# Last stage of a two-part kernel: a third PSUM buffer for h, the reciprocal in SBUF, and a loop of six blocks

## The chip, the cores and the metric

The kernel runs on one core of a Trainium2 chip. The metric is device time in microseconds, the median of several executions. Lower is better.

## What is computed

The program does two things one after the other. First a long convolution by Fourier transform, `y = irfft(rfft(x * v) * rfft(filter))`, whose result is gated as `x * y`. Then a wide layer with a rational activation on each of the 24,960 rows of that result (128 wide, 2,048 hidden):

```python
h = x @ w_in
P = a[0] + a[1] * h + a[2] * h**2 + a[3] * h**3
Q = 1.0 + abs(b[0]) * abs(h) + abs(b[1]) * h**2
out = (P / (Q + 1e-06)) @ w_out
```

All of it is float32. The change touches only the second part, which is the last stage of the kernel.

## The kernel before, in words

There are three stages. The first transforms `x * v` and the filter along one axis, the second multiplies the spectra and transforms back along the other, and the third, the last, unfolds the result, gates it with `x` and runs the wide layer.

The last stage goes over 30 blocks of 416 tokens for each of two batches. The unit of work is a step: one pair of hidden tiles, 2 x 128 hidden units by 416 tokens, so that most instructions work on 128 partitions by 832 elements. There are 16 steps to a block (`BLOCK_PAIRS`) and 480 in all. Every engine has its own order, written out by hand, and the engines meet only at semaphores. For step q it is:

- TensorE multiplies `g_s` of step q into `acc_p` (L878) and then makes h of step q+6 (`hidden`, L867, `LEAD_H = 6`) in one of two PSUM buffers `h_p`. A buffer is taken again when the numerator two steps earlier has been made.
- ScalarE takes the logarithm of the denominator of step q+1 (L669), the Exp of minus the logarithm of step q, which is the reciprocal and goes to the PSUM tensor `r_p` (L676), and for step q+4 the magnitude of h (L650, even steps only) and the square (L659).
- VectorE makes the magnitude of h of step q+4 on odd steps (L747), then `g_s` of step q out of numerator and reciprocal (`activation`, L785), then the numerator `num` of step q+4 out of the square and h (L752). Both of the last two are scalar_tensor_tensor instructions with two tensor inputs.
- GpSimd makes the denominator less its constant as `slope = mag * b1 + b0` (L617), then `den = slope * mag` (L625), both from SBUF to SBUF.

`num`, `square`, `mag`, `slope`, `den` and `g_s` lie in SBUF. `h_p`, `r_p`, `acc_p` and `m_p` are in PSUM: four banks for the two h buffers, two for `r_p`, one each for the others. The unfolding of the next block, its gating, its two transposes and the split of its values into a high and a low part go in between at the steps named in `UNFOLD`, `TIMES_X`, `TURN_IN`, `SPLIT_HI` and `SPLIT_LO`, all by way of the one bank `m_p`.

The loops are written so that the first and the last turn stand outside, and the turns between them are a hardware loop. A turn is two blocks (32 steps).

One instruction of the first stage matters for the argument. `product` on VectorE (L264, a tensor_tensor) multiplies `x_s` by `v_s`, both in SBUF, once in each of its 30 blocks, while GpSimd subtracts `uh_hi` from `uh` (L211, also a tensor_tensor, twice in each block):

```python
nc.vector.tensor_tensor(uh[:, s, :, 0:BD]..., x_s[:, s], v_s[:, s], ALU.mult)
nc.gpsimd.tensor_tensor(uh_lo[:, s, at], uh[:, s, at], uh_hi[:, s, at].bitcast(F32), ALU.subtract)
```

Other VectorE instructions of that stage that run beside L211 (L283, L285) take one tensor from PSUM (`g_p`) and one from SBUF (`part_s`).

Of the kernel before, what the change touches and what calls it, by code (L numbers as in the profile page):

```python
# [22 lines left out]
I32 = mybir.dt.int32  # L23
ALU = mybir.AluOpType
# [48 lines left out]
def hyena_mlp(nc, x, v, pos_emb, w1, w2, w_in, w_out, a, b, tab, out):  # L73
# [30 lines left out]
    with ExitStack() as whole:  # L104
# [420 lines left out]
        with ExitStack() as ctx:  # L525
# [50 lines left out]

            UNFOLD, TIMES_X, TURN_IN, SPLIT_HI, SPLIT_LO = (2, 6), (3, 7), (3, 7), (5, 9), (5, 9)
            SUMS, TURN_OUT, LEAVE = (0, 8), (0, 12), (2, 14)

            @block.sync  # L580
            def _(sp):
# [14 lines left out]
                load(1, 1)  # L596
                with sp.Fori(0, ITERS - 1) as i:
# [39 lines left out]
            def _(act):  # L637
# [7 lines left out]
                def magnitude(i, q):  # L645
                    G = i * PER + q
                    act.wait_ge(h_done, G + 1)
                    if positive(G - DEEP + 1):
                        act.wait_ge(den_done, G - DEEP + 1)
                    nc.scalar.activation(mag[:, q % DEEP], h_p[:, q % 2, :, 0:TOK], ACT.Abs).then_inc(mag_act, 1)  # L650

                def squared(i, q):
                    G = i * PER + q
                    act.wait_ge(h_done, G + 1)
                    if q % 2:
                        act.wait_ge(mag_dve, i * (PER // 2) + q // 2 + 1)
                    if positive(G - SQUARES + 1):
                        act.wait_ge(num_done, G - SQUARES + 1)
                    nc.scalar.activation(square[:, q % SQUARES], h_p[:, q % 2, :, 0:TOK], ACT.Square, bias=centre[:]  # L659
                                         ).then_inc(square_done, 1)  # L660
# [27 lines left out]
                def step(i, q, more, ahead):  # L688

                    blk, m = i * SLOTS + q // BLOCK_PAIRS, q % BLOCK_PAIRS  # L690
                    if ahead or q + 1 < PER:
# [24 lines left out]
                for q in range(PER):  # L716
                    step(ITERS - 1, q, q < BLOCK_PAIRS, q + LEAD_E < PER)
                c = J_BLOCKS * BATCH - 1
# [5 lines left out]
            def _(dve):  # L724
# [17 lines left out]
                def magnitude(i, q):  # L742
                    G = i * PER + q
                    dve.wait_ge(h_done, G + 1)
                    if positive(G - DEEP + 1):
                        dve.wait_ge(den_done, G - DEEP + 1)
                    nc.vector.tensor_scalar(mag[:, q % DEEP].bitcast(I32), h_p[:, q % 2, :, 0:TOK].bitcast(I32), NO_SIGN, None,  # L747
                                            ALU.bitwise_and).then_inc(mag_dve, 1)

                def numerator(i, q):  # L750
                    dve.wait_ge(square_done, i * PER + q + 1)
                    nc.vector.scalar_tensor_tensor(out=num[:, q % NUMS], in0=square[:, q % SQUARES], scalar=level[:],  # L752
                                                   in1=h_p[:, q % 2, :, 0:TOK], op0=ALU.add, op1=ALU.mult).then_inc(num_done, 1)

# [25 lines left out]
                def activation(i, q):  # L780
# [24 lines left out]
                def step(i, q, more, ahead):  # L805
                    blk, m = i * SLOTS + q // BLOCK_PAIRS, q % BLOCK_PAIRS
                    if m in SUMS:
# [7 lines left out]
                    def side():  # L815
                        nxt, s = (blk + 1) * 2, (q // BLOCK_PAIRS + 1) % SLOTS
                        if more and m in TIMES_X:
                            times_x(nxt + TIMES_X.index(m), i + (q // BLOCK_PAIRS + 1) // SLOTS, s, TIMES_X.index(m))
                        if more and m in SPLIT_LO:
                            split_lo(nxt + SPLIT_LO.index(m), s, SPLIT_LO.index(m))  # L820
# [12 lines left out]
                for q in range(PER):  # L833
                    step(ITERS - 1, q, q < BLOCK_PAIRS, q + LEAD_E < PER)
                sums(J_BLOCKS * BATCH - 1)

            @block.tensor
            def _(pe):
# [18 lines left out]
                def hidden(i, q):  # L857
                    G = i * PER + q
                    if q % BLOCK_PAIRS == 0:
                        pe.wait_ge(lo_done, (i * SLOTS + q // BLOCK_PAIRS + 1) * 2)  # L860
                    if positive(G - 1):
                        pe.wait_ge(num_done, G - 1)
                    s, b_ = q // BLOCK_PAIRS, q // PAIRS % BATCH
                    for t in range(2):
                        at = ((q % PAIRS) * 2 + t) * 128
                        for n, (w, f) in enumerate(((w_lo, xy_hi), (w_hi, xy_hi), (w_hi, xy_lo))):
                            mm = nc.tensor.matmul(h_p[:, q % 2, t, 0:TOK], w[:, at:at + 128], f[:, s, b_, :],  # L867
                                                  start=(n == 0), stop=(n == 2))
                    mm.then_inc(h_done, 1)

                def project(i, q):
                    G = i * PER + q
                    pe.wait_ge(act_done, G + 1)
                    if q % PAIRS == 0 and positive(G):
                        pe.wait_ge(oT_done, i * SLOTS * BATCH + q // PAIRS)
                    for t in range(2):
# [12 lines left out]
                def step(i, q, more, ahead):  # L889
                    blk, m = i * SLOTS + q // BLOCK_PAIRS, q % BLOCK_PAIRS  # L890
                    project(i, q)
# [3 lines left out]
                    if more and m in UNFOLD:  # L895
# [7 lines left out]

                        rows(nxt + half, i + (q // BLOCK_PAIRS + 1) // SLOTS, s, half, freed)
                    if more and m in TURN_IN:
# [26 lines left out]
                for q in range(PER):  # L932
                    step(ITERS - 1, q, q < BLOCK_PAIRS, q + LEAD_H < PER)
                turn_out(J_BLOCKS * BATCH - 1, lambda: pe.wait_ge(o_done, J_BLOCKS * BATCH - 1))
# [21 lines left out]
```

## Time and profile before

| | |
|---|---|
| median of 3 runs | 2239.24 us (2235.86 to 2241.52) |
| the profiled execution's own time | 2240.67 us |
| its span | 2238.9 us |
| TensorE busy | 2048.9 us, 92% |
| VectorE busy | 1805.7 us, 81% |
| ScalarE busy | 1822.0 us, 81% |
| GpSimd busy | 1894.0 us, 85% |
| first and last start of `den` (L625) | 675.1 and 2223.7 us |

The engines are PE (TensorE matmul), PEld (TensorE weight load), DVE (VectorE), ACT (ScalarE), POOL (GpSimd) and SP (the queue that issues the transfers). L625 is line 625 of the kernel. The last stage begins at about 645 us and fills the rest. Busy shares over the whole span mix three stages, so they are to be read stage by stage.

### The profile page before, as it was taken

To read this page: it belongs to the slowest core of one execution; us is meant where nothing else is said; L and a number is where in the kernel's file an instruction comes from. 1 tells how busy PE (TensorE), PEld (TensorE's weight loads), DVE (VectorE), ACT (ScalarE), POOL (GpSimd) and SP (SyncE) were. 2 spreads that over 40 slices of the span, in tenths; PEclk is the share of its full clock that TensorE was granted. 3 is DMA by queue.
4 is the path that set the end of the run, shared out by engine and by line. 5 is a ranking of instruction groups with operands and counts; after the bars stand their busy time and mean duration, and the time that the engine had idled before them with its cause. 6 is when DMAs were issued, how large, how long until landed. Compare 5 with 4: busy or idle time off the path is not lost. (4 is left out here: it accounts for less than half of the span.)

```text
span 2238.9 us, 33664 instructions
## 1 busy us (share of the span) xinstructions
PE 2048.9 (92%) x8964; PEld 1458.6 (65%) x8964; DVE 1805.7 (81%) x2271; ACT 1822.0 (81%) x2431; POOL 1894.0 (85%) x1218
## 2 busy tenths in 40 slices
PE   7888769999968999999999999999999999999997
PEld 5666559999955666666666666666666666666664
DVE  4777648888847888888888888888888888888887
ACT  4767646666638999999999999999999999899997
POOL 3666558888838999999999999999999999999997
PEclk9999979999979999999999999999999999999999
DMA  6888677666640111111111111111111111111100
GB/s 164 260 258 259 209 163 176 176 176 176 176 108 11 30 34 30 29 35 49 29 29 29 29 29 29 29 31 31 29 31 46 37 29 29 29 29 29 29 8 16
DMA packets 65724, 175.02 MB, mean 78 GB/s; under 512 B 5046, under 2 KB 8414, under 8 KB 62686
## 3 DMA queue, kind: packets, MB, share of 16 engines
q1 hardware_dynamic: 65694, 174.67, 29.4%
q8 instruction: 13, 0.21, 0.0%
q14 instruction: 17, 0.14, 0.0%
HBM read 102.89 MB, written 71.76 MB: 78 GB/s over the span
## 5 line engine op out<-in xcount | busy, mean ns | idle before, releaser
L625 POOL TENSOR_TENSOR den<-slope,mag 128x832 f32<-128x832 f32 x480 | 946.2, 1971 | 43.5 <-POOL slope L617 6.9
L878 PE MATMUL acc_p<-g_s,w_out_k 128*128 128x416 f32 x1920 | 784.1, 531 | 88.3 <-DVE g_s L785 83.5
L752 DVE SCALAR_TENSOR_TENSOR num<-square,level,h_p 128x832 f32<-128x832 f32 x480 | 517.8, 1079 | 90.1 <-ACT square L659 79.3
L617 POOL TENSOR_SCALAR slope<-mag,den_c 128x832 f32<-128x832 f32 x480 | 500.3, 1042 | 98.9 <-ACT mag L650 70.2
L785 DVE SCALAR_TENSOR_TENSOR g_s<-num,ratio,r_p 128x832 f32<-128x832 f32 x480 | 516.0, 1075 | 83.2 <-ACT r_p L676 54.6
L878 PEld LDWEIGHTS acc_p<-g_s,w_out_k 128*128 128x128 f32 x1920 | 332.6, 189 | 373.4 <-issue 221.8
L659 ACT ACTIVATE square<-h_p,centre 128x832 f32<-128x832 f32 x480 | 459.0, 956 | 128.7 <-DVE mag L747 112.5
L867 PE MATMUL h_p<-xy_hi,w_lo 128*128 128x416 f32 x960 | 459.1, 478 | 5.6 <-DVE num L752 4.3
L669 ACT ACTIVATE den<-den 128x832 f32<-128x832 f32 x480 | 431.1, 898 | 0.0
L676 ACT ACTIVATE r_p<-den 128x832 f32<-128x832 f32 x480 | 417.4, 870 | 12.9 <-DVE g_s L785 12.9
L867 PE MATMUL h_p<-xy_lo,w_hi 128*128 128x416 f32 x960 | 338.0, 352 | 0.0
L867 PE MATMUL h_p<-xy_hi,w_hi 128*128 128x416 f32 x960 | 337.5, 352 | 0.0
L867 PEld LDWEIGHTS h_p<-xy_hi,w_lo 128*128 128x128 f32 x960 | 181.6, 189 | 143.1 <-DVE num L752 113.0
L211 POOL TENSOR_TENSOR uh_lo<-uh,uh_hi 104x768 fp32r<-104x768 f32 x60 | 151.6, 2544 | 113.9 <-ACT uh_hi L239 113.8
L747 DVE TENSOR_SCALAR mag<-h_p 128x832 int32<-128x832 int32 x240 | 244.1, 1017 | 0.0
L409 POOL TENSOR_TENSOR bin_lo<-bin_s,bin_hi 120x768 fp32r<-120x768 f32 x96 | 178.3, 1858 | 71.2 <-ACT bin_hi L428 71.2
L867 PEld LDWEIGHTS h_p<-xy_hi,w_hi 128*128 128x128 f32 x960 | 182.4, 190 | 52.2 <-issue 51.4
L650 ACT ACTIVATE mag<-h_p 128x832 f32<-128x832 f32 x240 | 205.8, 857 | 3.2 <-PE h_p L867 3.2
L867 PEld LDWEIGHTS h_p<-xy_lo,w_hi 128*128 128x128 f32 x960 | 181.4, 189 | 1.4
L246 ACT ACTIVATE part_s<-g_p,turn_k 96x768 f32<-96x768 f32 x120 | 107.7, 898 | 83.0 <-PE g_p L333 83.0
L498 PE MATMUL x_p<-bin_hi,spread_lo 120*120 120x384 f32 x384 | 130.2, 339 | 28.5 <-POOL bin_lo L409 28.5
L498 PE MATMUL x_p<-bin_lo,spread_hi 120*120 120x384 f32 x384 | 130.6, 340 | 0.0
(79 smaller groups left out, 2805.4 us busy)
## 6 DMA issues: line engine op xcount, KB each, us to landing
bent<-bent_s SPq DMA_DIRECT2D x60, 576.0 KB, 4.8
bin_s<-bent SPq DMA_DIRECT2D x24, 1440.0 KB, 9.7
x_s<-in_x SPq DMA_DIRECT2D x60, 416.0 KB
back<-back_s SPq DMA_DIRECT2D x24, 960.0 KB, 7.8
vin_s<-back SPq DMA_DIRECT2D x30, 768.0 KB, 5.8
v_s<-in_v SPq DMA_DIRECT2D x30, 416.0 KB
out<-o_s SPq DMA_DIRECT2D x60, 208.0 KB
pos_s<-in_pos_emb SPq DMA_DIRECT2D x30, 88.0 KB
```

What stands on the lines that cost most here:

```text
L498: mm = nc.tensor.matmul(to, w, f, start=(n == 0), stop=(n == len(every) - 1))
L617: nc.gpsimd.tensor_scalar(slope[:, q % DEEP], mag[:, q % DEEP], den_c[:, 1:2], den_c[:, 0:1], ALU.mult, ALU.add).then_inc(slope_done, 1)
L625: nc.gpsimd.tensor_tensor(den[:, q % DEEP], slope[:, q % DEEP], mag[:, q % DEEP], ALU.mult).then_inc(den_done, 1)
L650: nc.scalar.activation(mag[:, q % DEEP], h_p[:, q % 2, :, 0:TOK], ACT.Abs).then_inc(mag_act, 1)
L659: nc.scalar.activation(square[:, q % SQUARES], h_p[:, q % 2, :, 0:TOK], ACT.Square, bias=centre[:]).then_inc(square_done, 1)
L669: nc.scalar.activation(den[:, q % DEEP], den[:, q % DEEP], ACT.Ln, bias=1.0 + EPS).then_inc(log_done, 1)
L676: nc.scalar.activation(r_p[:, :, 0:TOK], den[:, q % DEEP], ACT.Exp, scale=-1.0).then_inc(r_done, 1)
L747: nc.vector.tensor_scalar(mag[:, q % DEEP].bitcast(I32), h_p[:, q % 2, :, 0:TOK].bitcast(I32), NO_SIGN, None, ALU.bitwise_and).then_inc(ma ...
L752: nc.vector.scalar_tensor_tensor(out=num[:, q % NUMS], in0=square[:, q % SQUARES], scalar=level[:], in1=h_p[:, q % 2, :, 0:TOK], op0=ALU.a ...
L785: nc.vector.scalar_tensor_tensor(out=g_s[:, q % DEEP], in0=num[:, q % NUMS], scalar=ratio[:, 0:1], in1=r_p[:, :, 0:TOK], op0=ALU.add, op1= ...
L867: mm = nc.tensor.matmul(h_p[:, q % 2, t, 0:TOK], w[:, at:at + 128], f[:, s, b_, :], start=(n == 0), stop=(n == 2))
L878: mm = nc.tensor.matmul(acc_p[:, 0:TOK], w_out_k[:, ft], g_s[:, q % DEEP, t], start=(ft == 0), stop=(ft == FT - 1))
```

## The change

There are three h buffers in PSUM instead of two, and h is made seven steps ahead instead of six. The two banks that this takes come from `r_p`: the reciprocal now goes to `r_s`, an SBUF tensor with two buffers, so that the Exp of a step waits for the `g_s` of two steps earlier instead of that of the step before. A turn of the loop is six blocks instead of two (a multiple of the three h buffers), so there are 5 turns instead of 15. The second unfolding of a block, its gating, its turning and both splits each move one step earlier.

```diff
-            PER = SLOTS * BLOCK_PAIRS
-            ITERS = J_BLOCKS // SLOTS
-            LEAD_H, LEAD_E, DEEP, NUMS, SQUARES = 6, 4, 4, 8, 2
+            BLOCKS, TILES = 6, 3
+            PER = BLOCKS * BLOCK_PAIRS
+            ITERS = J_BLOCKS // BLOCKS
+            LEAD_H, LEAD_E, DEEP, NUMS, SQUARES = 7, 4, 4, 8, 2
...
+            r_s = sb("r_s", [128, 2, 2, TOK])
...
-            h_p = ps("h_p", [128, 2, 2, 512])
-            r_p = ps("r_p", [128, 2, 512])
+            h_p = ps("h_p", [128, TILES, 2, 512])
...
-            UNFOLD, TIMES_X, TURN_IN, SPLIT_HI, SPLIT_LO = (2, 6), (3, 7), (3, 7), (5, 9), (5, 9)
+            UNFOLD, TIMES_X, TURN_IN, SPLIT_HI, SPLIT_LO = (2, 5), (3, 6), (3, 6), (4, 8), (4, 8)
...
                 def reciprocal(i, q):
                     G = i * PER + q
                     act.wait_ge(log_done, G + 1)
-                    if positive(G):
-                        act.wait_ge(act_done, G)
-                    nc.scalar.activation(r_p[:, :, 0:TOK], den[:, q % DEEP], ACT.Exp, scale=-1.0).then_inc(r_done, 1)
+                    if positive(G - 1):
+                        act.wait_ge(act_done, G - 1)
+                    nc.scalar.activation(r_s[:, q % 2], den[:, q % DEEP], ACT.Exp, scale=-1.0).then_inc(r_done, 1)
...
                     nc.vector.scalar_tensor_tensor(out=g_s[:, q % DEEP], in0=num[:, q % NUMS], scalar=ratio[:, 0:1],
-                                                   in1=r_p[:, :, 0:TOK], op0=ALU.add, op1=ALU.mult).then_inc(act_done, 1)
+                                                   in1=r_s[:, q % 2], op0=ALU.add, op1=ALU.mult).then_inc(act_done, 1)
...
                 def hidden(i, q):
                     G = i * PER + q
...
-                    if positive(G - 1):
-                        pe.wait_ge(num_done, G - 1)
+                    if positive(G - TILES + 1):
+                        pe.wait_ge(num_done, G - TILES + 1)
```

The magnitude, the square and the numerator read `h_p[:, q % TILES]` instead of `h_p[:, q % 2]`. No instruction is added or removed in a step, and no shape is changed.

## Rows read from the trace of the kernel before

**Rows 1.** The page: busy time, share of the span and instructions of each engine.

```profile
PE 2048.9 (92%) x8964; PEld 1458.6 (65%) x8964; DVE 1805.7 (81%) x2271; ACT 1822.0 (81%) x2431; POOL 1894.0 (85%) x1218
```

**Rows 2.** Windows, last stage: window, length, busy PE, PEld, DVE, ACT, POOL, granted clock, DMA.

```profile
1500.00:1600.00 100.00, 94.83 (x359) 61.93 (x359) 85.66 (x89) 91.47 (x117) 92.61 (x63) 1.00 0.13 33
```

**Rows 3.** Groups of instructions, 760 us to the end: count, busy us, mean ns, idle before.

```profile
L625 POOL TENSOR_TENSOR den<-slope,mag 128x832 f32<-128x832 f32 x454 | 894.9, 1971 | 41.3 <-POOL slope L617 6.9
...
L785 DVE SCALAR_TENSOR_TENSOR g_s<-num,ratio,r_p 128x832 f32<-128x832 f32 x457 | 491.3, 1075 | 78.5 <-ACT r_p L676 51.3 <-issue 23.2
L752 DVE SCALAR_TENSOR_TENSOR num<-square,level,h_p 128x832 f32<-128x832 f32 x453 | 488.6, 1079 | 77.5 <-ACT square L659 67.4
L617 POOL TENSOR_SCALAR slope<-mag,den_c 128x832 f32<-128x832 f32 x453 | 472.2, 1042 | 63.1 <-ACT mag L650 35.6 <-DVE mag L747 21.6
...
L669 ACT ACTIVATE den<-den 128x832 f32<-128x832 f32 x455 | 408.7, 898 | 0.0
L676 ACT ACTIVATE r_p<-den 128x832 f32<-128x832 f32 x456 | 396.6, 870 | 12.6 <-DVE g_s L785 12.6
...
L747 DVE TENSOR_SCALAR mag<-h_p 128x832 int32<-128x832 int32 x226 | 229.8, 1017 | 0.0
```

**Rows 4.** One tile, `den`: GpSimd's 480 instructions, ns min/median/max, first and last start.

```profile
L625 POOL TENSOR_TENSOR den<-slope,mag x480: 1950/1972/1992, 675.1 to 2223.7; 128x832 f32<-128x832 f32 x160
```

**Rows 5.** Timeline, GpSimd: the longest wait of three blocks, one after another.

```profile
819.21 1.05 POOL L617 TENSOR_SCALAR slope<-mag,den_c 128x832 f32<-128x832 f32 x1 [0.77 <-DVE mag L747]
...
870.95 1.04 POOL L617 TENSOR_SCALAR slope<-mag,den_c 128x832 f32<-128x832 f32 x1 [0.76 <-DVE mag L747]
...
922.77 1.05 POOL L617 TENSOR_SCALAR slope<-mag,den_c 128x832 f32<-128x832 f32 x1 [0.77 <-DVE mag L747]
```

**Rows 6.** Waits of GpSimd, 800 to 1000 us: total us, times, longest.

```profile
POOL slope L617 <- ACT mag L650: 4.9, 11, 0.6
POOL slope L617 <- DVE mag L747: 3.1, 4, 0.8
```

**Rows 7.** Timeline, GpSimd: two steps with nothing to wait for, and one longer gap.

```profile
689.38 1.03 POOL L617 TENSOR_SCALAR slope<-mag,den_c 128x832 f32<-128x832 f32 x1
...
692.46 1.04 POOL L617 TENSOR_SCALAR slope<-mag,den_c 128x832 f32<-128x832 f32 x1
...
784.81 1.98 POOL L625 TENSOR_TENSOR den<-slope,mag 128x832 f32<-128x832 f32 x1 [0.16 <-POOL slope L617]
```

**Rows 8.** Timeline, first stage: L264 and L211, apart and together.

```profile
17.03 1.21 DVE L264 TENSOR_TENSOR uh<-x_s,v_s 104x1024 f32<-104x1024 f32 x1
18.42 1.81 POOL L211 TENSOR_TENSOR uh_lo<-uh,uh_hi 104x768 fp32r<-104x768 f32 x1 [16.68 <-ACT uh_hi L239]
...
38.52 3.29 POOL L211 TENSOR_TENSOR uh_lo<-uh,uh_hi 104x768 fp32r<-104x768 f32 x1 [6.96 <-ACT uh_hi L239]
...
189.70 5.12 POOL L211 TENSOR_TENSOR uh_lo<-uh,uh_hi 104x768 fp32r<-104x768 f32 x2 [3.03 <-ACT uh_hi L239]
...
190.10 1.21 DVE L264 TENSOR_TENSOR uh<-x_s,v_s 104x1024 f32<-104x1024 f32 x1
```

**Rows 9.** Tile `uh_lo`, single GpSimd instructions that L264 falls into: ns min/median/max.

```profile
L211 POOL TENSOR_TENSOR uh_lo<-uh,uh_hi x1: 3324/3324/3324, 189.7 to 189.7; 104x768 fp32r<-104x768 f32 x1
...
L211 POOL TENSOR_TENSOR uh_lo<-uh,uh_hi x1: 3416/3416/3416, 197.9 to 197.9; 104x768 fp32r<-104x768 f32 x1
```

**Rows 10.** Timeline of one step, from a `den` to the next `slope`.

```profile
772.14 1.97 POOL L625 TENSOR_TENSOR den<-slope,mag 128x832 f32<-128x832 f32 x1
...
773.61 1.07 DVE L785 SCALAR_TENSOR_TENSOR g_s<-num,ratio,r_p 128x832 f32<-128x832 f32 x1
...
774.10 1.04 POOL L617 TENSOR_SCALAR slope<-mag,den_c 128x832 f32<-128x832 f32 x1
```

**Rows 11.** Windows, columns as in rows 2: a sparse stretch, and one after idleness.

```profile
0.00:20.00 20.00, 6.59 (x21) 3.46 (x22) 3.40 (x4) 4.56 (x8) 2.77 (x7) 1.00 0.71 166
...
655.00:660.00 5.00, 3.01 (x4) 1.01 (x4) 0.00 (x0) 0.27 (x1) 0.00 (x0) 0.50 1.00 224
```

More of the change, by code:

```diff
@@ L596, in _ @@
                 load(1, 1)
-                with sp.Fori(0, ITERS - 1) as i:
+                with sp.Fori(0, J_BLOCKS // SLOTS - 1) as i:
                     for s in range(SLOTS):
@@ L649, in magnitude @@
                         act.wait_ge(den_done, G - DEEP + 1)
-                    nc.scalar.activation(mag[:, q % DEEP], h_p[:, q % 2, :, 0:TOK], ACT.Abs).then_inc(mag_act, 1)
+                    nc.scalar.activation(mag[:, q % DEEP], h_p[:, q % TILES, :, 0:TOK], ACT.Abs).then_inc(mag_act, 1)
                 def squared(i, q):
@@ L658, in squared @@
                         act.wait_ge(num_done, G - SQUARES + 1)
-                    nc.scalar.activation(square[:, q % SQUARES], h_p[:, q % 2, :, 0:TOK], ACT.Square, bias=centre[:]
+                    nc.scalar.activation(square[:, q % SQUARES], h_p[:, q % TILES, :, 0:TOK], ACT.Square, bias=centre[:]
                                          ).then_inc(square_done, 1)
@@ L688, in step @@
                 def step(i, q, more, ahead):
-                    blk, m = i * SLOTS + q // BLOCK_PAIRS, q % BLOCK_PAIRS
+                    blk, m = i * BLOCKS + q // BLOCK_PAIRS, q % BLOCK_PAIRS
                     if ahead or q + 1 < PER:
@@ L716, in _ @@
                 for q in range(PER):
-                    step(ITERS - 1, q, q < BLOCK_PAIRS, q + LEAD_E < PER)
+                    step(ITERS - 1, q, q < PER - BLOCK_PAIRS, q + LEAD_E < PER)
                 c = J_BLOCKS * BATCH - 1
@@ L805, in step @@
                 def step(i, q, more, ahead):
-                    blk, m = i * SLOTS + q // BLOCK_PAIRS, q % BLOCK_PAIRS
+                    blk, m = i * BLOCKS + q // BLOCK_PAIRS, q % BLOCK_PAIRS
                     if m in SUMS:
@@ L817, in side @@
                         if more and m in TIMES_X:
-                            times_x(nxt + TIMES_X.index(m), i + (q // BLOCK_PAIRS + 1) // SLOTS, s, TIMES_X.index(m))
+                            times_x(nxt + TIMES_X.index(m), i * (BLOCKS // SLOTS) + (q // BLOCK_PAIRS + 1) // SLOTS, s, TIMES_X.index(m))
                         if more and m in SPLIT_LO:
@@ L833, in _ @@
                 for q in range(PER):
-                    step(ITERS - 1, q, q < BLOCK_PAIRS, q + LEAD_E < PER)
+                    step(ITERS - 1, q, q < PER - BLOCK_PAIRS, q + LEAD_E < PER)
                 sums(J_BLOCKS * BATCH - 1)
@@ L859, in hidden @@
                     if q % BLOCK_PAIRS == 0:
-                        pe.wait_ge(lo_done, (i * SLOTS + q // BLOCK_PAIRS + 1) * 2)
-                    if positive(G - 1):
-                        pe.wait_ge(num_done, G - 1)
-                    s, b_ = q // BLOCK_PAIRS, q // PAIRS % BATCH
+                        pe.wait_ge(lo_done, (i * BLOCKS + q // BLOCK_PAIRS + 1) * 2)
+                    if positive(G - TILES + 1):
+                        pe.wait_ge(num_done, G - TILES + 1)
+                    s, b_ = q // BLOCK_PAIRS % SLOTS, q // PAIRS % BATCH
                     for t in range(2):
@@ L866, in hidden @@
                         for n, (w, f) in enumerate(((w_lo, xy_hi), (w_hi, xy_hi), (w_hi, xy_lo))):
-                            mm = nc.tensor.matmul(h_p[:, q % 2, t, 0:TOK], w[:, at:at + 128], f[:, s, b_, :],
+                            mm = nc.tensor.matmul(h_p[:, q % TILES, t, 0:TOK], w[:, at:at + 128], f[:, s, b_, :],
                                                   start=(n == 0), stop=(n == 2))
@@ L874, in project @@
                     if q % PAIRS == 0 and positive(G):
-                        pe.wait_ge(oT_done, i * SLOTS * BATCH + q // PAIRS)
+                        pe.wait_ge(oT_done, i * BLOCKS * BATCH + q // PAIRS)
                     for t in range(2):
@@ L889, in step @@
                 def step(i, q, more, ahead):
-                    blk, m = i * SLOTS + q // BLOCK_PAIRS, q % BLOCK_PAIRS
+                    blk, m = i * BLOCKS + q // BLOCK_PAIRS, q % BLOCK_PAIRS
                     project(i, q)
@@ L902, in freed @@
                                 pe.wait_ge(o_done, blk * BATCH)
-                        rows(nxt + half, i + (q // BLOCK_PAIRS + 1) // SLOTS, s, half, freed)
+                        rows(nxt + half, i * (BLOCKS // SLOTS) + (q // BLOCK_PAIRS + 1) // SLOTS, s, half, freed)
                     if more and m in TURN_IN:
@@ L932, in _ @@
                 for q in range(PER):
-                    step(ITERS - 1, q, q < BLOCK_PAIRS, q + LEAD_H < PER)
+                    step(ITERS - 1, q, q < PER - BLOCK_PAIRS, q + LEAD_H < PER)
                 turn_out(J_BLOCKS * BATCH - 1, lambda: pe.wait_ge(o_done, J_BLOCKS * BATCH - 1))
```

4 lines of the change are left out of this document (2 added, 2 removed).

## Prediction

> **What bounds the kernel now.** I read the page first, then windows of 100 us. On the page GpSimd is third in share with 85% [rows 1], which says nothing, because it mixes three stages. In a window of the last stage four engines stand between 86% and 95% [rows 2]: TensorE 94.8, GpSimd 92.6, ScalarE 91.5, VectorE 85.7 of 100 us. TensorE's matmuls overlap in the pipeline, so its 94.8 is a ceiling of its work.
>
> Which engine sets the pace is seen from what one step costs on each. The long wait of GpSimd comes back once a block, at 819.21, 870.95 and 922.77 us [rows 5]: 51.74 and 51.82 us apart, 16 steps each, so a step takes 3.236 us. Over the stage, the 480 starts of `den` go from 675.1 to 2223.7 [rows 4]: 1548.6 us for 479 intervals, 3.233 us each. On GpSimd a step has one `slope` of 1.042 and one `den` of 1.971 us [rows 3], 3.013 together, and where it waits for nothing, slope follows slope after 692.46 - 689.38 = 3.08 us [rows 7]. So 3.08 of 3.24 us are GpSimd's own work. What is left is its waits for a magnitude from ScalarE or VectorE, 4.9 + 3.1 us in 200 us [rows 6], 4%. GpSimd is the bound, with little waits in between that the other engines cause in the steps in which they also prepare the next block. The most that any reordering can give back is 3.233 - 3.08 = 0.15 us a step, 479 x 0.15 = 73 us. Anything that lengthens GpSimd's work is paid at once, 480 times over.
>
> **The change part by part.**
>
> *Third h buffer, lead of seven.* On TensorE, h of step q+6 waited for the numerator of step q+4; now h of step q+7 waits for the numerator of step q+4. The wait is the same, but its product is a step earlier than its readers. What this can remove is part of the waits of [rows 6]. They come from magnitudes late on ScalarE and VectorE, whose own groups show no idle time before the magnitude (0.0 for L747) [rows 3], so most of it is queueing behind other work on these two engines and not a late h. From -73 us to 0 by itself, and 0 if GpSimd becomes slower for another reason, because then nobody is late for it.
>
> *Exp into SBUF with two buffers.* The wait of the Exp for `g_s`, 12.6 us in the stage [rows 3], goes. The Exp itself took 870 ns into PSUM; the nearest row with its output in SBUF is the logarithm with 898 ns [rows 3]. That is 0.03 us a step on ScalarE, which has 100 - 91.5 us of room in 100 [rows 2]: nothing, and if it had no room it would be 480 x 0.03 = 14 us.
>
> *Second block's preparation one step earlier, loop of six blocks.* The same instructions in another place. The back edge of the loop comes every second block; the two intervals of [rows 5], of which one holds a back edge, differ by 0.08 us, so 10 back edges fewer are worth 1 us. The other side is a body three times as long on each engine, which the trace of before doesn't show. I bound it by the longest wait of a block, 0.8 us [rows 6], per back edge: 2 us. Both taken as nothing. No DMA is added or moved past another; SP's queue has the same order.
>
> *`g_s` now reads both of its tensors from SBUF.* This is the part that decides. The instruction keeps its engine, form and size, so VectorE's own 1.075 us [rows 3] should stay. But what it does to GpSimd is to be read in the first stage. There VectorE's L264 has two SBUF inputs. Alone it takes 1.21 us (17.03), and L211 on GpSimd, alone, 1.81 us (18.42) [rows 8]. Once they overlap, L264, which starts 0.4 us after GpSimd's instruction, still takes 1.21 us (190.10), but the pair of L211 takes 5.12 us instead of 2 x 1.81 [rows 8]. The single instruction that L264 falls into takes 3.324 or 3.416 us [rows 9]; 28 of the 30 L264 fall into one (the two at the start don't), and the shortest so lengthened has 3.29 us [rows 8]. So 1.21 us of VectorE's reading cost GpSimd 3.324 - 1.81 = 1.51 to 3.416 - 1.81 = 1.61 us. VectorE lost nothing. The second L211 of each pair, beside which run instructions with one input in PSUM and one in SBUF, is not lengthened (5.12 - 3.32 = 1.80). In the last stage `g_s` and `num` have one of each so far, and not one of 480 `den` took longer than 1.992 us against a median of 1.972 [rows 4], although VectorE is busy 86% of the time. So it is the second SBUF input that counts.
>
> The Trainium skill (SBUF — State Buffer, Who interferes with whom) says that a VectorE instruction with two SBUF inputs contends with a GpSimd instruction that reads SBUF, and one with at most one does not. By that, the trace agrees with which forms collide. It also says that the one that starts first keeps the shared ports for its whole length and the other blocks fully. There the trace differs: GpSimd's instruction had started first and was the one that was lengthened. By that rule of the Trainium skill, with the two instructions excluding each other and nothing on top, the sum would be 2687 us (the first rival has it from rows).
>
> Price per step. Of the 1.51 to 1.61 us, 1.21 are the VectorE instruction and 0.30 to 0.40 come on top. With `g_s` at 1.075 us the charge is 1.075 + 0.30 to 0.40 = 1.38 to 1.48 us if what comes on top is fixed, and 1.075 x 1.25 to 1.33 = 1.34 to 1.43 if it goes in proportion. I take 1.40. It is charged wherever `g_s` lies on GpSimd's work, and GpSimd has no gaps to speak of. In a slower step the places also lock: the logarithm starts when a `den` ends, the Exp after it, and `g_s` after that, some 0.9 + 0.9 us behind the end of that `den` [rows 3]; the next `den` starts 1.1 us behind it (1.04 `slope` and a gap) and lasts 1.97 us, so `g_s` begins 0.7 us into it, all of it inside, as L264 was in L211. Today it lies partly in `den` and partly in `slope` (773.61 beside 772.14 and 774.10) [rows 10].
>
> *Sum.* GpSimd's unstalled step is 3.08 [rows 7]. The idle time before `den` is 41.3 us for 454 of them, 0.09 each [rows 3], because some have a gap of 0.16 [rows 7]; 3.013 + 0.09 gives the 3.10 that I take. Of 480 `g_s`, all but the four or so at either end fall on GpSimd's work: 476. New distance from first to last `den`: 479 x 3.10 + 476 x 1.40 = 1484.9 + 666.4 = 2151.3 us, against 1548.6 before [rows 4]: +602.7 us. The step becomes 4.50 us. The other engines have at most 94.8% of 3.236 = 3.07 us of work in it (TensorE; ScalarE 2.96, VectorE 2.77) [rows 2], so none of them is bound, and nothing of the three h buffers' gain is left, since GpSimd waits for nobody. The profiled execution's 2240.67 us become 2843; the median is 1.4 us below that execution, so 2842 us.
>
> **The rivals.** Changes below 0.3% (7 us) can't be told from none in this kernel.
>
> *Collision without the extra.* The two exclude each other, whoever waits, and nothing comes on top: 479 x 3.10 + 476 x 1.075 = 1996.6, +448, so 2687 us. VectorE would be the one that waits: its `g_s` would start only at the end of a `den`, and the next `slope` behind it. The Trainium skill has this in the section named above. Against it: the 28 lengthened L211, both sizes with 0.3 us or more on top. For it: L264 is a tensor_tensor and `g_s` a scalar_tensor_tensor, which may hold the ports differently.
>
> *No collision, faster.* If the scalar_tensor_tensor form doesn't read its second input in the way that collides with GpSimd, what remains is a better fed GpSimd: at best 479 x 3.08 = 1475.3, -73 us, 2166 us, and with half the waits gone 2203 us. For it: no row shows this form with two SBUF inputs beside GpSimd. Against it: L264 has the same two full tensor reads. It decides below a charge of 0.15 us a step, where waits removed and charge are equal.
>
> *Nothing to be seen.* The form doesn't collide, and the waits in GpSimd are VectorE's and ScalarE's queueing, which the change leaves: 2232 to 2246 us.
>
> *TensorE falls to the lower clock.* At 4.50 us a step TensorE is busy at most 3.07, 68%. The granted clock was 0.50 (1.2 GHz) in a stretch that followed idleness, and 1.00 (2.4 GHz) in one with 6.59 us of work in 20 [rows 11]. If it were halved throughout, TensorE's step would be up to 6.1 us and the bound: 479 x 6.1 - 1548.6 = +1373, over 3600 us. But a TensorE that is the bound is busy all the time, which speaks against its staying low. Taken part of the time, it lies between 2930 and 3200.
>
> **How the numbers follow.** Collision as in the first stage: 0.74, 2842 us, its own range 2785 (charge 1.28, that is 0.2 on top) to 2900 (charge 1.48 and a step of 3.14). Collision without the extra: 0.13, 2687 us. TensorE's clock or a charge that compounds: 0.05, above 2930. No collision, faster: 0.05. Nothing: 0.03. The range that holds 8 in 10 reaches down to the second case with the shortest step, 479 x 3.08 + 476 x 1.075 = 1987.0, +438, and up to a step of 3.013 + 0.16 = 3.17 with the highest charge, 479 x 3.17 + 476 x 1.48 = 2222.9, +674: 2675 to 2915. Slower: 0.74 + 0.13 + 0.05 = 0.92; same 0.03; faster 0.05.
>
> **What would show it.** In the changed kernel `den` (L625 or near it) should have a mean near 3.3 to 3.4 us instead of 1.97, with `slope` as before, or the two together near 4.4; `g_s` should stay near 1.07 us; GpSimd should be busy over 97% of each window of the last stage, with no waits for a magnitude; ScalarE, VectorE and TensorE near 65% with idle time behind `den` and what follows from it. If instead `g_s` waits and `den` stays at 1.97 us, it is the first rival. If `den` stays at 1.97 us and GpSimd's waits in [rows 6] shrink, it is the faster case. The prediction is wrong by size if part of `g_s` falls on `slope` and is charged otherwise there.

## The result, and the profile after

The changed kernel takes 2540.41 us (2539.63 to 2545.92), the kernel before 2237.78 us in the same comparison: a ratio of 1.135, 95% interval 1.1335 to 1.1372. It is 303 us slower. The direction was forecast; the forecast of 2842 us was not met, since it had twice the loss, and the time lies below the stated range.

The page of the changed kernel, span and busy time:

```profile
span 2544.1 us, 32808 instructions
...
PE 2093.0 (82%) x8964; PEld 1506.6 (59%) x8964; DVE 2110.7 (83%) x2271; ACT 1854.4 (73%) x2431; POOL 2261.8 (89%) x1218
```

One window of its last stage, with the columns of [rows 2]:

```profile
1500.00:1600.00 100.00, 81.72 (x301) 53.51 (x300) 92.98 (x77) 79.03 (x99) 97.83 (x52) 0.98 0.13 31
```

GpSimd is at 97.8% and everybody else has room; VectorE's busy time went up from 85.7 to 93.0 although it did fewer instructions (77 instead of 89), because its records now hold time in which it stands. The granted clock of TensorE is 0.98, close to its upper level of 2.4 GHz. From 800 to 900 us it is 0.93, and GpSimd is at 97.83 of 100 us there as well: TensorE isn't what the kernel waits for.

Groups of the last stage (760 to 2500 us), to be held against [rows 3]:

```profile
L626 POOL TENSOR_TENSOR den<-slope,mag 128x832 f32<-128x832 f32 x451 | 973.6, 2159 | 38.6 <-POOL slope L618 2.0
L786 DVE SCALAR_TENSOR_TENSOR g_s<-num,ratio,r_s 128x832 f32<-128x832 f32 x450 | 802.5, 1783 | 83.0 <-issue 61.9 <-DVE num L753 12.5 <-ACT r_s L677 7.1
...
L618 POOL TENSOR_SCALAR slope<-mag,den_c 128x832 f32<-128x832 f32 x450 | 735.2, 1634 | 2.8 <-issue 2.8
L753 DVE SCALAR_TENSOR_TENSOR num<-square,level,h_p 128x832 f32<-128x832 f32 x450 | 481.9, 1071 | 28.1 <-ACT square L660 27.0
...
L670 ACT ACTIVATE den<-den 128x832 f32<-128x832 f32 x450 | 403.3, 896 | 135.3 <-POOL den L626 130.4
L677 ACT ACTIVATE r_s<-den 128x832 f32<-128x832 f32 x450 | 398.4, 885 | 0.0
```

Three instructions changed. `g_s` went from 1.075 to 1.783 us, `slope` from 1.042 to 1.634, `den` from 1.971 to 2.159. `num`, whose inputs still are one of SBUF and one of PSUM, kept its 1.07. The Exp went from 0.870 to 0.885. GpSimd no longer waits for a magnitude, and ScalarE waits for GpSimd instead (130.4 us before L670).

The tiles `den` and `slope` of the whole stage, ns min/median/max and first and last start, against [rows 4]:

```profile
L618 POOL TENSOR_SCALAR slope<-mag,den_c x480: 1028/1808/1911, 677.2 to 2529.2; 128x832 f32<-128x832 f32 x160
L626 POOL TENSOR_TENSOR den<-slope,mag x480: 1938/1976/3418, 678.4 to 2530.3; 128x832 f32<-128x832 f32 x160
```

479 intervals of `den` in 2530.3 - 678.4 = 1851.9 us: 3.866 us a step instead of 3.233, +303.3 us. That is the whole loss.

Where within a step it goes, the timeline of the changed kernel shows (start us, length us). First the usual case:

```profile
1513.41 1.98 POOL L626 TENSOR_TENSOR den<-slope,mag 128x832 f32<-128x832 f32 x1
...
1513.63 2.64 DVE L786 SCALAR_TENSOR_TENSOR g_s<-num,ratio,r_s 128x832 f32<-128x832 f32 x1 [0.23 <-DVE num L753]
...
1515.37 1.81 POOL L618 TENSOR_SCALAR slope<-mag,den_c 128x832 f32<-128x832 f32 x1
```

`g_s` begins 0.22 us after a `den` that then takes its normal 1.98 us, to 1515.39. `g_s` ends at 1516.27, 0.88 us behind the end of `den`: it stood still until then. And `slope`, which begins at 1515.37, takes 1.81 instead of 1.04 us. So here VectorE waited for GpSimd, and then GpSimd's next instruction waited for VectorE, 0.77 us. Of the 480 `slope` of the stage 362 are lengthened like that, to 1.8 us in the mean; this is the bulk of the loss. The other order occurs too: 61 `den` take 2.81 to 2.85 us, 42 take 2.52 to 2.76, and 9 take 3.41. One of the nine:

```profile
762.42 0.68 DVE L732 TENSOR_TENSOR xy<-m_p,x_s 104x512 f32<-104x512 f32 x1
762.50 3.41 POOL L626 TENSOR_TENSOR den<-slope,mag 128x832 f32<-128x832 f32 x1
...
763.02 1.07 DVE L786 SCALAR_TENSOR_TENSOR g_s<-num,ratio,r_s 128x832 f32<-128x832 f32 x1
```

`g_s` directly follows `xy` on VectorE, takes its normal 1.07 us to 764.09, and `den` ends at 765.91, 1.82 us after that. `den` has lost 1.44 us, of which 0.5 us passed before `g_s` is recorded as running. That is close to the 1.40 us of the prediction, in 9 steps of 480. It is L264 and L211 of [rows 8] again: L264 ended at 190.10 + 1.21 = 191.31 and L211 at 189.70 + 3.32 = 193.02, 1.71 us later; in the pair of the second size it is 1.71 us too (L264 at 198.41, L211 from 197.91 for 3.416). The two sizes of [rows 9] are two starting distances, 0.40 and 0.50 us, and not two prices.

### The profile page after: what moved, and what is told of

Read it like the earlier page. It is cut to its first block and busy times, and to the rows that moved or that the text cites. A ratio compares the mean times of both kernels' runs of the same rounds, so it can differ in the third digit from the quotient of the medians.

```text
span 2544.1 us, 32808 instructions
## 1 busy us (share of the span) xinstructions
PE 2093.0 (82%) x8964; PEld 1506.6 (59%) x8964; DVE 2110.7 (83%) x2271; ACT 1854.4 (73%) x2431; POOL 2261.8 (89%) x1218
## 5 line engine op out<-in xcount | busy, mean ns | idle before, releaser
L879 PE MATMUL acc_p<-g_s,w_out_k 128*128 128x416 f32 x1920 | 820.0, 551 | 351.5 <-DVE g_s L786 348.4
L626 POOL TENSOR_TENSOR den<-slope,mag 128x832 f32<-128x832 f32 x480 | 1038.6, 2164 | 41.0 <-POOL slope L618 2.0
L786 DVE SCALAR_TENSOR_TENSOR g_s<-num,ratio,r_s 128x832 f32<-128x832 f32 x480 | 850.6, 1772 | 93.3 <-issue 65.4
L618 POOL TENSOR_SCALAR slope<-mag,den_c 128x832 f32<-128x832 f32 x480 | 779.4, 1624 | 36.6 <-ACT mag L651 32.6
L879 PEld LDWEIGHTS acc_p<-g_s,w_out_k 128*128 128x128 f32 x1920 | 343.6, 195 | 654.2 <-DVE g_s L786 429.4
L670 ACT ACTIVATE den<-den 128x832 f32<-128x832 f32 x480 | 430.0, 896 | 146.2 <-POOL den L626 141.2
L868 PE MATMUL h_p<-xy_hi,w_lo 128*128 128x416 f32 x960 | 507.4, 529 | 5.1 <-DVE num L753 3.2
L677 ACT ACTIVATE r_s<-den 128x832 f32<-128x832 f32 x480 | 425.0, 886 | 0.0
L211 POOL TENSOR_TENSOR uh_lo<-uh,uh_hi 104x768 fp32r<-104x768 f32 x60 | 151.7, 2544 | 117.9 <-ACT uh_hi L239 117.7
L868 PEld LDWEIGHTS h_p<-xy_hi,w_lo 128*128 128x128 f32 x960 | 188.9, 197 | 89.8 <-DVE num L753 60.0
L868 PEld LDWEIGHTS h_p<-xy_hi,w_hi 128*128 128x128 f32 x960 | 189.3, 197 | 80.4 <-issue 79.7
L283 DVE SCALAR_TENSOR_TENSOR bent_s<-g_p,turn_k,part_s 96x384 f32<-96x384 f32 x120 | 73.5, 612 | 74.5 <-ACT part_s L246 74.5
```

The source lines that it names most:

```text
L618: nc.gpsimd.tensor_scalar(slope[:, q % DEEP], mag[:, q % DEEP], den_c[:, 1:2], den_c[:, 0:1], ALU.mult, ALU.add).then_inc(slope_done, 1)
L626: nc.gpsimd.tensor_tensor(den[:, q % DEEP], slope[:, q % DEEP], mag[:, q % DEEP], ALU.mult).then_inc(den_done, 1)
L670: nc.scalar.activation(den[:, q % DEEP], den[:, q % DEEP], ACT.Ln, bias=1.0 + EPS).then_inc(log_done, 1)
L677: nc.scalar.activation(r_s[:, q % 2], den[:, q % DEEP], ACT.Exp, scale=-1.0).then_inc(r_done, 1)
L868: mm = nc.tensor.matmul(h_p[:, q % TILES, t, 0:TOK], w[:, at:at + 128], f[:, s, b_, :], start=(n == 0), stop=(n == 2))
L879: mm = nc.tensor.matmul(acc_p[:, 0:TOK], w_out_k[:, ft], g_s[:, q % DEEP, t], start=(ft == 0), stop=(ft == FT - 1))
```

## The experiments

**One part alone: the reciprocal in SBUF.** Kernel before, with `r_s` and its two buffers and nothing else of the change:

```diff
-                    if positive(G):
-                        act.wait_ge(act_done, G)
-                    nc.scalar.activation(r_p[:, :, 0:TOK], den[:, q % DEEP], ACT.Exp, scale=-1.0).then_inc(r_done, 1)
+                    if positive(G - 1):
+                        act.wait_ge(act_done, G - 1)
+                    nc.scalar.activation(r_s[:, q % 2], den[:, q % DEEP], ACT.Exp, scale=-1.0).then_inc(r_done, 1)
...
-                                                   in1=r_p[:, :, 0:TOK], op0=ALU.add, op1=ALU.mult).then_inc(act_done, 1)
+                                                   in1=r_s[:, q % 2], op0=ALU.add, op1=ALU.mult).then_inc(act_done, 1)
```

> The kernel before with one thing of the change alone: the reciprocal in SBUF with two buffers, so that g_s reads both tensors from SBUF. Two h buffers, lead six, loop of two blocks and all places as before. Theory (turns at the port): in the changed kernel slope has a mean of 1.62 instead of 1.04 us and den 2.16 instead of 1.97, together 0.78 us a step, and GpSimd waits for nobody; all of it comes from g_s. Then this kernel has it too: a step of about 3.87 us, 2525 to 2560 us. Rival (the third buffer, the loop of six or the moved places cost part of it): clearly less than 2520 us, and slope and den closer to their old means.

Measured: 2540.15 us, ratio 1.134 (1.131 to 1.138), the time of the whole change. Its groups from 760 to 2230 us:

```profile
L625 POOL TENSOR_TENSOR den<-slope,mag 128x832 f32<-128x832 f32 x382 | 790.3, 2069 | 34.8 <-POOL slope L617 5.9
L785 DVE SCALAR_TENSOR_TENSOR g_s<-num,ratio,r_s 128x832 f32<-128x832 f32 x382 | 735.4, 1925 | 48.4 <-issue 39.1 <-ACT r_s L676 8.1 <-DVE num L752 0.3
L617 POOL TENSOR_SCALAR slope<-mag,den_c 128x832 f32<-128x832 f32 x382 | 653.8, 1711 | 0.0
```

`slope` and `den` are 3.780 us together, 0.77 above the 3.013 of before. The split between the two differs from that in the changed kernel (of all 480, 409 `slope` are lengthened here and only 2 `den` take 3.41), the sum (3.79 there) hardly does. This one edit is the whole loss.

**Half a dose.** Kernel before, reciprocal of odd steps in SBUF, of even steps in PSUM:

```diff
-                    nc.scalar.activation(r_p[:, :, 0:TOK], den[:, q % DEEP], ACT.Exp, scale=-1.0).then_inc(r_done, 1)
+                    nc.scalar.activation(r_s[:, 0] if q % 2 else r_p[:, :, 0:TOK], den[:, q % DEEP], ACT.Exp, scale=-1.0).then_inc(r_done, 1)
...
-                                                   in1=r_p[:, :, 0:TOK], op0=ALU.add, op1=ALU.mult).then_inc(act_done, 1)
+                                                   in1=r_s[:, 0] if q % 2 else r_p[:, :, 0:TOK], op0=ALU.add, op1=ALU.mult).then_inc(act_done, 1)
```

> The kernel before, with the reciprocal of the odd steps in SBUF (one buffer) and that of the even steps in PSUM as before. Theory: every g_s with two SBUF inputs costs GpSimd 0.78 us, and the charge is paid out of GpSimd's waits of 0.15 us a step first. 3.09 + 0.39 = 3.48 us a step, so +118 us, 2355 us; up to 2425 us if the waits are not absorbed. Rival (once there is a collision at all the order of the engines is upset): close to the full loss, over 2450 us.

Measured: 2351.69 us, ratio 1.050 (1.047 to 1.053). Its tile `g_s`, the two forms of one instruction in one run, and its `den` and `slope` (the first from the tile `den`, the second a group from 760 to 2230 us):

```profile
L786 DVE SCALAR_TENSOR_TENSOR g_s<-num,ratio,r_p x240: 1064/1073/1084, 682.6 to 2338.5; 128x832 f32<-128x832 f32 x120
L786 DVE SCALAR_TENSOR_TENSOR g_s<-num,ratio,r_s x240: 1083/2188/2464, 686.1 to 2340.7; 128x832 f32<-128x832 f32 x120
...
L626 POOL TENSOR_TENSOR den<-slope,mag x480: 1937/1976/1995, 671.5 to 2334.2; 128x832 f32<-128x832 f32 x160
...
L618 POOL TENSOR_SCALAR slope<-mag,den_c 128x832 f32<-128x832 f32 x424 | 603.0, 1422 | 0.0
```

The 240 with a PSUM input never took over 1.084 us, the 240 with two SBUF inputs took 2.188 in the median. No `den` is lengthened here, so the charge is all in `slope`: 1.422 instead of 1.042 in the mean, 0.38 us a step or 0.77 for each colliding `g_s`. GpSimd's step without waits, 3.08 us [rows 7], and 0.385 give 3.465; the measured step is (2334.2 - 671.5) / 479 = 3.471. The loss is 113 us, against 118 expected.

**GpSimd writes and doesn't read.** The changed kernel, with

```diff
-                    nc.gpsimd.tensor_scalar(slope[:, q % DEEP], mag[:, q % DEEP], den_c[:, 1:2], den_c[:, 0:1], ALU.mult,
-                                            ALU.add).then_inc(slope_done, 1)
+                    nc.gpsimd.memset(slope[:, q % DEEP], 1.0).then_inc(slope_done, 1)
...
-                    nc.gpsimd.tensor_tensor(den[:, q % DEEP], slope[:, q % DEEP], mag[:, q % DEEP], ALU.mult).then_inc(den_done, 1)
+                    pool.sem_inc(pool_passed, 1)
+                    nc.gpsimd.memset(den[:, q % DEEP], 1.0).then_inc(den_done, 1)
```

> The changed kernel, but both GpSimd instructions of a step only write: slope and den are filled with ones, their arithmetic is left out. Theory (VectorE and GpSimd take turns for a shared way to read SBUF): g_s goes back from 1.77 to about 1.07 us although it still reads two tensors from SBUF. Rival (two SBUF inputs are slow for VectorE by themselves, or what is shared is the writing): g_s stays at 1.5 us or more. The time is no measure here, since GpSimd's work is another.

Tile `g_s` and one window:

```profile
L786 DVE SCALAR_TENSOR_TENSOR g_s<-num,ratio,r_s x480: 1072/1083/1087, 684.3 to 2265.2; 128x832 f32<-128x832 f32 x160
...
1500.00:1600.00 100.00, 92.60 (x351) 60.65 (x350) 84.59 (x88) 90.01 (x114) 48.42 (x62) 1.00 0.13 31
```

`g_s` takes 1.083 us in the median and never over 1.087, with two SBUF inputs and beside a GpSimd that writes half of the time. What the two engines take turns for is reading SBUF. The time, 2274.61 us in one run, held a surprise: with GpSimd half idle the kernel still was 1.5% slower than before. The loop of six and the moved places, below, take 2273.69 us by themselves.

**Who has the turn.** Kernel before, one wait more in the first stage. `turned[0]` is raised by the L285 right ahead of L264, so L264 can't be sent while L285 runs:

```diff
                         dve.wait_ge(uh_lo_done, (blk - 1) * 2)
+                        dve.wait_ge(turned[0], (blk - 2) * 2 + 1)
                     nc.vector.tensor_tensor(uh[:, s, :, 0:BD]...
```

> The kernel before, with one wait more in the first stage: L264 waits for the VectorE instruction ahead of it (L285) to finish, so that it can't be sent to the engine while that one still runs. Theory (turns are taken in the order of sending, and an instruction that waits behind its predecessor already holds the turn): GpSimd's L211, which starts some 0.4 us earlier, now has the turn: it keeps its 1.81 us, L264 is recorded with about 2.4 us instead of 1.21, and the second L211 is lengthened by about 1 us. Rival (the prediction's reading: VectorE's two SBUF reads always run at full rate and GpSimd pays them with 0.3 us on top): L264 stays at 1.21 and the first L211 at 3.3 us.

Its timeline (the lines have moved by one, L265 is the L264 of before):

```profile
182.77 0.60 DVE L286 SCALAR_TENSOR_TENSOR bent_s<-g_p,turn_k,part_s 96x384 f32<-96x384 f32 x1
182.88 1.82 POOL L211 TENSOR_TENSOR uh_lo<-uh,uh_hi 104x768 fp32r<-104x768 f32 x1 [5.42 <-ACT uh_hi L239]
183.41 2.38 DVE L265 TENSOR_TENSOR uh<-x_s,v_s 104x1024 f32<-104x1024 f32 x1
184.87 2.58 POOL L211 TENSOR_TENSOR uh_lo<-uh,uh_hi 104x768 fp32r<-104x768 f32 x1 [0.17 <-ACT uh_hi L239]
```

The roles are exchanged, as the theory of turns had it. GpSimd's instruction keeps 1.82 us, VectorE's goes from 1.21 to 2.38 and ends 1.09 us behind GpSimd's end at 184.70; the second L211 is lengthened to 2.58. In [rows 8] the record of L264 begins at a similar distance, 0.4 us behind that of L211, and GpSimd paid. What the edit changes is only that L264 can no longer be sent while its predecessor is running. So in the first stage an L264 that stood queued behind L285 already had the turn, though its record starts later. (The time, 2283.17 us in one run, is that of a first stage with a wait in it, in which the granted clock was 0.90 from 100 to 200 us and 0.87 from 200 to 280 us; it isn't read further.)

Standing queued isn't enough in general, as the last stage of the changed kernel shows. There 27 `g_s` directly follow an `xy` and start 0.52 to 0.60 us into a `den`. In 9 of them `den` pays, as at 762.50 above; in the other 18 `g_s` waits:

```profile
1073.42 0.68 DVE L732 TENSOR_TENSOR xy<-m_p,x_s 104x512 f32<-104x512 f32 x1
1073.50 1.98 POOL L626 TENSOR_TENSOR den<-slope,mag 128x832 f32<-128x832 f32 x1
...
1074.02 2.34 DVE L786 SCALAR_TENSOR_TENSOR g_s<-num,ratio,r_s 128x832 f32<-128x832 f32 x1
```

**The rest of the change without the collision.** The changed kernel with the reciprocal in PSUM. There is no room for this beside three h buffers of two banks, so an h buffer is one bank here, written by both halves and read twice; half of the hidden units are left out of the result. The magnitudes and the square read it with the same `to_broadcast`:

```diff
-            h_p = ps("h_p", [128, TILES, 2, 512])
+            h_p = ps("h_p", [128, TILES, 1, 512])
+            r_p = ps("r_p", [128, 2, 512])
...
-                            mm = nc.tensor.matmul(h_p[:, q % TILES, t, 0:TOK], w[:, at:at + 128], f[:, s, b_, :],
+                            mm = nc.tensor.matmul(h_p[:, q % TILES, 0, 0:TOK], w[:, at:at + 128], f[:, s, b_, :],
...
-                                                   in1=h_p[:, q % TILES, :, 0:TOK], op0=ALU.add, op1=ALU.mult).then_inc(num_done, 1)
+                                                   in1=h_p[:, q % TILES, :, 0:TOK].to_broadcast([128, 2, TOK]), op0=ALU.add, op1=ALU.mult).then_inc(num_done, 1)
```

> The changed kernel with the reciprocal back in PSUM (one buffer, the old wait), and with three h buffers, lead seven, loop of six and the new places kept. To make room, an h buffer is one bank: both halves of the pair are written to the same bank and that bank is read twice, so half of the hidden units are left out of the result; all instructions keep their sizes. Theory: no g_s collides any more, the means of slope and den are 1.04 and 1.97 us, and the time shows what the rest of the change is worth, between 2166 (all GpSimd waits gone) and 2238 us. Rival (the rest costs something): over 2245 us.

Its control is the kernel before with the same one-bank form:

> Control for the run with the one-bank h buffers: the kernel before, two h buffers, with both halves of a pair written to one bank and that bank read twice (half of the hidden units left out of the result). Every theory: as before, within 0.3%, 2231 to 2245 us. If not, the one-bank form has a price of its own and the other run is read against this one.

Measured: control 2241.11 us, ratio 1.001 (0.999 to 1.002), so the form has no price. The rest of the change: 2272.32 us, ratio 1.014 (1.011 to 1.017). I had expected a gain or nothing and got a loss. `g_s`, `slope` and `den` are as before (1.076, 1.037, 1.969 us), and GpSimd waits more. Its waits from 800 to 1800 us, total us, times, longest, first in the kernel before and then in this one:

```profile
POOL slope L617 <- ACT mag L650: 24.8, 58, 0.6
POOL slope L617 <- DVE mag L747: 14.7, 19, 0.8
...
POOL slope L618 <- DVE mag L748: 42.5, 59, 1.3
POOL slope L618 <- ACT mag L651: 18.2, 74, 0.8
```

Three more runs split that loss, and a fourth tried to turn it round.

**Loop and places, without third buffer and lead.** The changed kernel with two h buffers, lead six and the reciprocal in PSUM:

```diff
-            BLOCKS, TILES = 6, 3
-            LEAD_H, LEAD_E, DEEP, NUMS, SQUARES = 7, 4, 4, 8, 2
+            BLOCKS, TILES = 6, 2
+            LEAD_H, LEAD_E, DEEP, NUMS, SQUARES = 6, 4, 4, 8, 2
```

> The kernel before with the loop of six blocks and the new places of the second unfolding, gating, turning and splits; two h buffers, lead six and the reciprocal in PSUM as before. The run without collision but with all the rest of the change took 2272 us, 34 us over the kernel before, and GpSimd waited in it three or four times a block for VectorE's magnitude. Theory (the moved places queue on VectorE and ScalarE): most of it is here, 2260 to 2280 us. Rival (the lead of seven or the third buffer costs it): 2231 to 2245 us.

Measured: 2273.69 us, ratio 1.015 (1.013 to 1.017).

**The loop alone.** The same with the old places:

```diff
-            UNFOLD, TIMES_X, TURN_IN, SPLIT_HI, SPLIT_LO = (2, 5), (3, 6), (3, 6), (4, 8), (4, 8)
+            UNFOLD, TIMES_X, TURN_IN, SPLIT_HI, SPLIT_LO = (2, 6), (3, 7), (3, 7), (5, 9), (5, 9)
```

> As the run with loop and places, but with the old places: the loop of six blocks alone. Theory: the longer body costs some us at the four points where a turn begins, 2238 to 2252 us. Rival (the loop is the cost, not the places): 2260 us or more.

Measured: 2246.50 us, ratio 1.0020 (1.0006 to 1.0034). The loop costs about 4 us (1 to 8), under the 0.3% that the prediction took as the least that can be told. The places are the cost: 1.015 against 1.002, 27 us.

**Third buffer and lead seven at the old places.** As the run with three h buffers of one bank, with the places line just shown:

> Three h buffers of one bank, lead seven, loop of six blocks, reciprocal in PSUM, and the places of the second unfolding, gating, turning and splits as in the kernel before (half of the hidden units left out of the result, as in the run with the new places that took 2272 us). The loop of six alone took 2246 us. Theory (a late h is not what anybody waits for): 2240 to 2252 us. Rival (the third buffer gives its gain only where the places don't queue): under 2235 us.

Measured: 2242.02 us, ratio 1.0022 (1.0006 to 1.0039), the same as the loop alone. The third buffer gives nothing at either set of places, in the one-bank form; with two banks and without the collision it was not run.

**Other places.** Kernel before, with the extra work of VectorE put into the steps in which it makes no magnitude, and of ScalarE likewise:

```diff
-            UNFOLD, TIMES_X, TURN_IN, SPLIT_HI, SPLIT_LO = (2, 6), (3, 7), (3, 7), (5, 9), (5, 9)
-            SUMS, TURN_OUT, LEAVE = (0, 8), (0, 12), (2, 14)
+            UNFOLD, TIMES_X, TURN_IN, SPLIT_HI, SPLIT_LO = (2, 6), (4, 8), (4, 8), (5, 9), (6, 10)
+            SUMS, TURN_OUT, LEAVE = (0, 8), (0, 12), (1, 13)
```

> The kernel before with other places only: gating on VectorE at steps 4 and 8 instead of 3 and 7, turning at 4 and 8, splits on VectorE at 6 and 10 instead of 5 and 9, so that VectorE does them in steps in which it makes no magnitude, and the copy of the result on ScalarE at 1 and 13 instead of 2 and 14, where ScalarE makes none. Theory (GpSimd's waits of 2.5 us a block are queueing behind such work): a part of them goes, 2190 to 2225 us. Rival (they come from the chain through m_p): within 0.5% of before.

Measured: 2338.42 us, ratio 1.043 (1.040 to 1.045). A clear miss: GpSimd's waits, 800 to 1800 us, grew to

```profile
POOL slope L617 <- ACT mag L650: 66.1, 109, 1.3
POOL slope L617 <- DVE mag L747: 33.6, 72, 0.9
```

Which of its four moved entries (`TIMES_X`, `TURN_IN`, `SPLIT_LO`, `LEAVE`) does the harm was not taken apart.

**Is GpSimd the bound before the change?** Kernel before, with the two memsets of the run above in place of GpSimd's arithmetic:

> The kernel before, with GpSimd's two instructions of a step only writing ones (0.79 us each as in the same edit of the changed kernel, so 1.6 instead of 3.0 us a step); their arithmetic is left out. The prediction says that GpSimd is the bound of the last stage. If so, the stage falls to what the next engine allows, 3.07 us a step at most on TensorE: under 2165 us. Rival (the order of VectorE, ScalarE and TensorE sets the step of 3.24 us, and GpSimd with 3.08 us of work only fits into it; the changed kernel with this edit still took 2275 us): 2225 to 2245 us, as before.

Measured: 2239.77 us, ratio 1.0001 (0.9985 to 1.0017). One window:

```profile
1500.00:1600.00 100.00, 94.87 (x360) 61.99 (x359) 85.36 (x90) 91.42 (x117) 48.49 (x62) 1.00 0.13 33
```

GpSimd's work was halved and nothing changed. It was not the bound.

**VectorE's copy of the sums behind `g_s`.** Kernel before, with one block of its step moved:

```diff
-                    if m in SUMS:
-                        c = blk * BATCH + SUMS.index(m) - 1
-                        if positive(c + 1):
-                            sums(c)
                     if ahead and (q + LEAD_E) % 2:
                         magnitude(i + (q + LEAD_E) // PER, (q + LEAD_E) % PER)
                     activation(i, q)
+                    if m in SUMS:
+                        c = blk * BATCH + SUMS.index(m) - 1
+                        if positive(c + 1):
+                            sums(c)
```

> The kernel before, with VectorE copying acc_p to oT behind g_s of its step instead of ahead of it. VectorE waited 0.8 us there twice a block for TensorE's last product. Theory: that idle time goes, but TensorE's first product of the next group waits for the copy, 0.6 us later; net between -20 and +10 us. Rival (TensorE sets the pace): slower by 15 to 40 us.

Measured: 2207.50 us, ratio 0.985 (0.983 to 0.987): 33 us faster than before, more than I expected, and the only kernel here that beats it. Its tile `den`, and the waits of TensorE that it creates (800 to 2200 us), below them the wait of VectorE in the kernel before (same stretch), which is gone here:

```profile
L625 POOL TENSOR_TENSOR den<-slope,mag x480: 1949/1972/1990, 680.2 to 2198.6; 128x832 f32<-128x832 f32 x160
...
PEld acc_p L878 <- DVE oT L793: 17.7, 25, 0.7
...
PE acc_p L878 <- DVE oT L793: 10.3, 28, 0.6
...
DVE oT L793 <- PE acc_p L878: 42.0, 54, 0.9
```

The step is (2198.6 - 680.2) / 479 = 3.170 us instead of 3.233. VectorE's idle time at the copy, 42.0 us, was part of what set the pace of the old kernel; TensorE's new waits for it, 28.0 us together, cost less.

## Why the prediction was right and wrong

*What bounds the kernel: wrong.* I took GpSimd for the bound because its 3.08 us were nearest to the step of 3.24. With its work halved the time stayed at 2240 us. What is left is the hand-written order of the other three engines, in which GpSimd's 3.08 us just fitted. GpSimd's waits were a sign of that, and I had read them as small disturbances of a bound engine. That moving one block on VectorE took 33 us off agrees with it, but which of the three sets most of the step stays open. For the sum this changed nothing, because above 3.24 us GpSimd is the bound: in the changed kernel it is busy 97.8%, and freeing it there brings 2540 back to 2275 us.

*Third buffer, lead of seven: right.* I had said that a late h is not what anybody waits for. Two runs with it give 1.014 and 1.0022, their counterparts without it 1.015 and 1.0020.

*Exp with two buffers into SBUF: right.* 885 instead of 870 ns, hidden.

*Places and loop "taken as nothing": right only under the collision.* By themselves the places cost 27 us and the loop about 4. In the changed kernel GpSimd's longer step hides both, so the reciprocal alone gives the time of the whole.

*Collision: right in kind.* The second SBUF input of `g_s` is what costs, the PSUM form of the same instruction in the same kernel doesn't, and it is paid once per `g_s`.

*Its price: the step that failed.* "Price per step" put it at 1.40 us for each `g_s`: 1.075 for the instruction and 0.30 to 0.40 "on top", with every `g_s` inside a `den` "as L264 was in L211". It is 2.164 + 1.624 - 3.013 = 0.775 us in the changed kernel (means of `den` and `slope` over all 480), 0.77 in the reciprocal alone, and 1.422 + 1.976 - 3.013 = 0.385 in the half dose, 0.77 for each colliding `g_s`. With it the prediction's own sum gives 479 x 3.10 + 476 x 0.775 = 1853.8 us; measured are 1851.9. (The price is from the same run, so this says only that no other term is missing.) Two things were misread. What came on top in [rows 8] was no fixed price of overlapping; it was time during which L211 was recorded and stood, before L264's own record began. The last stage has that arrangement too, and there the price is the predicted one, 1.44 us, but only for 9 of 480 `den`; the prediction took it for every step. And in the usual case, where `den` goes first, GpSimd isn't charged with the recorded length of `g_s`. In the step shown `slope` starts at 1515.37, `g_s` ends at 1516.27, and `slope` ends 0.91 us later, 0.13 less than its usual 1.04: it stands for 0.90 us and gets 0.13 back, which is the 0.77. What it does in these 0.13 us no run shows.

*Who waits: wrong.* I expected `g_s` to stay at 1.07 us and `den` to grow to 3.3. Mostly `g_s` waits (1.78 us in the mean) and `slope` grows. I had weighed the rule that the one which starts first keeps the ports and the other blocks fully, and had set it aside, because in [rows 8] GpSimd's record starts first and GpSimd is lengthened. The Trainium skill (SBUF — State Buffer, Who interferes with whom) puts it by issue: "Issue order, not op shape, decides who blocks." The run with the extra wait agrees with it: 1.82 and 2.38 us with the roles exchanged. I had read the start of a record as the issue, which it doesn't show; in the last stage the same recorded distances went both ways. The first rival had this mechanism, `g_s` waiting and the next `slope` behind it, at a chance of 0.13, but with the full 1.075 us, which gave 2687; it, too, was 150 us too slow.

## What to carry to other kernels

Before a tile is moved from PSUM to SBUF, count the SBUF inputs of every VectorE instruction that reads it: one with two takes turns with GpSimd's reads, here 0.77 us for 832 elements, and a GpSimd near its limit pays every one. An engine with the highest sum of work per step need not be the bound; taking half of its work away is one run, and tells. And where two records overlap and one is longer, measure from end to end (1.71 us in both sizes) before subtracting lengths, and count how many steps have the arrangement that the price was read from (here 9 of 480).

## What the runs showed of the hardware

- VectorE with two SBUF inputs and GpSimd reading SBUF exclude each other, and either can be the one that waits. With GpSimd first, the 832-element `g_s` ends 0.88 us behind GpSimd's end and the next GpSimd instruction is 0.77 us longer.
- A VectorE instruction that stands queued behind its predecessor can already hold GpSimd up: the 28 L264 that fall into an L211 did it, none did once a wait kept them from being queued (no L211 over 2.64 us), and 9 `den` lost 1.44 us to a `g_s` of 1.07. In 18 other cases, with recorded distances of 0.52 to 0.60 us instead of 0.52, it didn't, so a record's start doesn't tell who goes first.
- GpSimd's memsets don't collide with it (`g_s` at most 1.087 us), nor does VectorE with one SBUF and one PSUM input (at most 1.084 us in the same kernel that had 2.19 for the other form).
